# RWKV-like attention, gated MLP and a routed MLP in one kernel: the weighing of a token's own value is moved from GpSimd to VectorE and ScalarE

## The reference, cut to what matters

```python
# attention: batch 4, 8 heads, 768 tokens, head size 48
for t in range(S):
    cur = einsum('bhd,bhe->bhde', u * k[t], v[t])          # the token's own contribution, weight u
    y[:, :, t] = einsum('bhd,bhde->bhe', r[t], state + cur)
    state = w * state + einsum('bhd,bhe->bhde', k[t], v[t])
x = y as (3072 tokens, 384)
# first MLP
h = x @ w_in                                               # 384 -> 2048
g = where(h >= 1, h, where(h <= -1, 0, (h + 1) ** 2 / 4))
x = g @ w_out                                              # 2048 -> 384
# routed MLP: 8 experts, 384 -> 1024 -> 384, top 1 by cosine logits
```

## Time and profile before

| | |
|---|---|
| median of 3 runs | 806.8 us (805.24 to 806.94) |
| profiled execution | 806.01 us, span 804.3 us |
| PE busy | 739.9 us, 92% of the span |
| DVE busy | 425.6 us, 53% |
| ACT busy | 304.3 us, 38% |
| POOL busy | 149.6 us, 19% |

### The profile page before, as it was taken

The page is one execution under the profiler, slowest core; times in us unless marked ns, Lnnn a source line. Parts: engine busy times, 40 slices in busy tenths (PEclk is TensorE's granted clock), DMA queues, the critical chain, the costliest instruction groups (busy, mean ns, idle before and its releaser), DMA issues. The chain is left out here.

```text
span 804.3 us, 12788 instructions
## 1 busy us (share of the span) xinstructions
PE 739.9 (92%) x4978; PEld 619.3 (77%) x4979; DVE 425.6 (53%) x677; ACT 304.3 (38%) x505; POOL 149.6 (19%) x170
## 2 busy tenths in 40 slices
PE   3789898999999999999999999999359999999995
PEld 2668687788877887788878888888249999998985
DVE  6778765575647565475746564544354323223232
ACT  2546443543445343544444443644233212122120
POOL 7433531222222211122222200000060000000000
PEclk9999988999999999999999999999769999999998
DMA  8792110211121111111110000000360202202021
GB/s 150 197 226 48 20 30 11 70 30 21 30 69 31 31 30 22 59 30 31 28 43 1 1 1 30 11 1 1 106 212 1 79 0 79 79 1 78 0 78 39
DMA packets 88316, 40.36 MB, mean 50 GB/s; under 512 B 77112, under 2 KB 84928, under 8 KB 88256
## 3 DMA queue, kind: packets, MB, share of 16 engines
q1 hardware_dynamic: 86800, 34.61, 17.2%
q10 hardware_dynamic: 1456, 4.93, 1.6%
HBM read 30.10 MB, written 9.44 MB: 49 GB/s over the span
## 5 line engine op out<-in xcount | busy, mean ns | idle before, releaser
L856 PE MATMUL x_ps<-g_p,wout_hi 128*128 128x512 f32 x576 | 186.7, 405 | 3.5 <-DVE g_p L672 3.4
L870 PE MATMUL h_ps<-x0T,win_hi 128*128 128x512 f32 x576 | 180.1, 394 | 1.2 <-DVE x0T L601 1.2
L472 ACT ACTIVATE above<-h_ps,minus_one 128x512 f32<-128x512 f32 x96 | 65.9, 687 | 196.4 <-DVE mid L681 196.4
L681 DVE TENSOR_SCALAR mid<-h_ps 128x512 f32<-128x512 f32 x96 | 66.2, 690 | 124.7 <-PE h_ps L870 124.5
L856 PEld LDWEIGHTS x_ps<-g_p,wout_hi 128*128 128x128 f32 x576 | 104.4, 190 | 32.3 <-DVE g_p L672 6.5
L870 PEld LDWEIGHTS h_ps<-x0T,win_hi 128*128 128x128 f32 x576 | 107.5, 189 | 24.4 <-DVE x0T L601 1.5
L1401 PE MATMUL ch_ps<-x_p,w_p 128*128 128x512 f32 x432 | 109.2, 400 | 11.9 <-DVE w_p L1467 11.9
L685 DVE TENSOR_TENSOR mid<-mid,above 128x512 f32<-128x512 f32 x96 | 82.6, 861 | 70.0 <-ACT mid L473 70.0
L856 PE MATMUL x_ps<-g_p,wout_lo 128*128 128x512 f32 x288 | 113.2, 393 | 0.0
L870 PE MATMUL h_ps<-x0T,win_lo 128*128 128x512 f32 x288 | 112.6, 391 | 0.0
L1390 PE MATMUL cy_ps<-w_p,h_p 128*128 128x384 f32 x576 | 107.7, 336 | 0.0
(11 more groups left out here) (208 smaller groups left out, 652.1 us busy)
## 6 DMA issues: line engine op xcount, KB each, us to landing
xr<-xT_scratch SPq DMA_DIRECT2D x8, 768.0 KB, 4.7
rkv<-in_r SPq DMA_DIRECT2D x24, 192.0 KB, 3.0
rkv<-in_k SPq DMA_DIRECT2D x24, 192.0 KB, 3.4
rkv<-in_v SPq DMA_DIRECT2D x24, 192.0 KB, 2.8
xT_scratch<-xbuf ACTq DMA_DIRECT2D x6, 768.0 KB, 3.3
out<-acc SPq DMA_DIRECT2D x12, 384.0 KB, 2.4
win_raw<-in_moe_w_in SPq DMA_DIRECT2D x48, 64.0 KB, 2.7
wout_raw<-in_moe_w_out SPq DMA_DIRECT2D x4, 768.0 KB, 6.3
```

The source lines that it names most:

```text
L472: raises(act.activation(above[:, f % 2], h_ps[f % 2][:, :], ACT.Relu, bias=minus_one[:, :]), "over")
L681: raises(dve.tensor_scalar(mid[:, f % NM], h_ps[f % 2][:, :], -1.0, 1.0, ALU.max, ALU.min), "clamped")
L856: last = pe.matmul(x_ps[kk][:, :], (wout_hi, wout_lo)[a][:, f, cols], g_p[:, f % NG, b], start=(f == 0 and n == 0), stop=(f == NF1 - 1 and ...
L870: last = pe.matmul(h_ps[f % 2][:, :], (win_hi, win_lo)[a][:, f // QF, kk, cols], x0T[:, c % 2, b, kk], start=(kk == 0 and n == 0), stop=(k ...
```

## The change

For tiles 4 to 23 the two products of `own_weight` are issued by DVE, between `scale_k` and `own_sum`, and the diagonals by ACT, as 8 copies of 128x128 for each tile in place of one POOL instruction of 128x1024. Four of the 8 copies stand behind `g_hi` at f % 4 = 3 of the step before the tile's first, the other four behind `g_hi` at f % 4 = 0. For tile 4 all eight stand behind `g_hi` of step 0 of chunk 0. POOL keeps the copies of v and its three subtractions of weights, with nothing ahead of them but the copies of v.

```diff
         def diagonal_here(eng, it):
-            if it in (1, 3):
-                wait(eng, "diag_act", it // 2)
+            if it in (0, 2):
+                wait(eng, "diag_done", it // 2)
             elif it >= 0:
-                wait(eng, "diag_done", it // 2 if it < B else it - 2)
+                wait(eng, "diag_act", it // 2 if it < B else it - 2)
+        def own_products(eng, it, to):
+            src = rkv[:, it % B]
+            raises(eng.tensor_tensor(to[:, :, :], src[:, 0], u_rep[:, :, :], ALU.mult), "ru_done")
+            wait(eng, "ru_done", it)
+            raises(eng.tensor_tensor(to[:, :, :], to[:, :, :], src[:, 1], ALU.mult), "ruk_done")
...
                 for it in range(B, NTILE):
-                    own_weight(it, ruk)
                     rest_of_v(it, vz[:, it % 2])
-                    own_diagonal(it)
                     if it == B + 2:
...
-                def own_diagonal(it):
+                def own_diagonal(it, heads=range(H)):
                     wait(act, "q_ready", it)
-                    for h in range(H):
-                        last = act.activation(first[it].sc_m[:, h], ident[:, :], ACT.Copy, scale=q[:, it, h:h + 1])
-                    raises(last, "diag_act")
+                    if it >= B:
+                        wait(act, "y_done", it - 1)
+                    for h in heads:
+                        last = act.activation(tile_set(it).sc_m[:, h], ident[:, :], ACT.Copy, scale=q[:, it % B, h:h + 1])
+                    if H - 1 in heads:
+                        raises(last, "diag_act")
...
                         raises(act.activation(g_p[:, f % NG, 0], mid[:, f % NM], ACT.Copy), "g_hi")
+                        if attn and f % 4 == 0:
+                            own_diagonal(it, range(H // 2 if f or c else 0, H))
+                        if f % 4 == 3 and it + 1 < NTILE:
+                            own_diagonal(it + 1, range(H // 2))
                         if c == 0 and f == 1:
                             split_win(1)
...
+                def own_weight(it):
+                    rk_here(dve, it)
+                    wait(dve, "q_ready", it - 1)
+                    own_products(dve, it, ruk)
...
                 scale_k(B)
+                own_weight(B)
                 own_sum(B)
...
                             scale_k(it + 1)
+                            own_weight(it + 1)
                             own_sum(it + 1)
```

More of the change, by code:

```diff
@@ L350, in own_weight @@
                     rk_here(pool, it)
-                    if it >= B:
-                        wait(pool, "q_ready", it - 1)
-                    src = rkv[:, it % B]
-                    raises(pool.tensor_tensor(to[:, :, :], src[:, 0], u_rep[:, :, :], ALU.mult), "ru_done")
-                    wait(pool, "ru_done", it)
-                    raises(pool.tensor_tensor(to[:, :, :], to[:, :, :], src[:, 1], ALU.mult), "ruk_done")
+                    own_products(pool, it, to)
                 def rest_of_v(it, dst):
@@ L369, in own_diagonal @@
                     wait(pool, "q_ready", it)
-                    if it >= B:
-                        wait(pool, "y_done", it - 1)
                     raises(pool.tensor_tensor(tile_set(it).sc_m[:, :, :],
```

## The result

| | before | after |
|---|---|---|
| median (lowest to highest) | 806.0 us (805.0 to 806.9, 4 runs) | 815.2 us (811.8 to 818.6, 4 runs) |
| profiled execution | 806.01 us, span 804.3 | 811.77 us, span 810.0 |
| PE / DVE / ACT / POOL busy | 739.9 / 425.6 / 304.3 / 149.6 us | 736.8 / 422.7 / 348.3 / 59.2 us |

The ratio is 1.0125, 95% interval 1.0081 to 1.0169: slower by 9.2 us, forecast +9.8 (816.6, within the range). In what follows a "fall" is a drop of TensorE's granted clock from 1.00 towards 0.50. A window of 4 us that shows a value between them is a mean over both.

What follows compares the result with a forecast made beforehand. PE was taken as almost full and setting the end, so only its waits count. Terms 4.7 + 3.6 + 1.8 + 0.2 gave +10.3 on 806.01, so 816.3, plus 0.3: 816.6 us, range 811 to 821.

Steps and rivals of the forecast that it cites:

- Term 1: End of chunks 0 to 3: the last down waits longer for DVE's low part, +1.17 us four times, +4.7.
- Term 2: First tile of chunks 1 to 4: ACT's second four copies delay above and the update, +0.91 us four times, +3.6.
- Term 3: Steps 3 to 5 of chunks 1 to 4: kT comes late for the scores, +0.45 us four times, +1.8.
- Term 4: Chunk 0: four pieces and a half-counted kept clock, sum +0.2 us, between -3.5 and +4.
- Steps 0 and 1: Chunk 0: lateness of 1.17 us and 8 copies fill ACT's idle time around g_hi, +0.3 to +0.5 us.
- Step 4: Chunk 0: like Term 3, but a weight piece's split stands in place of the square, +1.3 us.
- The race: Chunk 0: POOL's first subtraction against DVE's state update; +1.3 us if POOL first, -0.2 if DVE, middle +0.5.
- The third wait: Chunk 0: wait of 3.16 us splits into two of about 1.3; g_sum earlier -0.5, half a kept clock -1.5.
- Rival A: With POOL silent, chunk 0's long waits shrink and TensorE keeps its clock, -12.8 us there: 803.3; 5%.
- Rival B: Only the chunk's end counts, ACT's copies fit its idle time, terms 2 and 3 near zero: 811.3 us; 13%.
- Rival C: Chunk 0 goes badly: POOL wins, clock falls all three times and another, +4 to +7: 821 to 823 us; 12%.
- Rival D: Longer waits at chunk starts lower the clock in each of four chunks, 3 us each: 828.6 us; 5%.

Runs made afterwards that it cites:

- e4: The changed kernel run once more, unaltered: 815.4 us, ratio 1.0127.
- e1: The kernel before with only the two products of tiles 4 to 23 moved to DVE, diagonals left on POOL: 814.3 us, ratio 1.0113.
- e3: The changed kernel with DVE taking the low part of step 15 ahead of the scaling, products and q: 809.9 us, ratio 1.0054.
- e2: The changed kernel with the two products given back to POOL, so only the diagonals are moved, to ACT: 801.3 us, ratio 0.9955.
- e9: The changed kernel with ACT's square of step 3 put ahead of the four copies of that step, chunks 1 to 5: 816.3 us, ratio 1.0134.
- e5: The changed kernel with POOL's first subtraction in chunk 0 held until DVE's low part of tile 5's rows is done: 814.3 us, ratio 1.0127.
- e6: The changed kernel with two more DVE products in step 15, lengthening the wait at chunk ends: 822.6 us, ratio 1.0228.
- e8: e2 with the low part first in step 15 and the second four copies of a chunk's first tile moved behind ACT's output copies: 797.6 us, ratio 0.9907.
- e7: The kernel before with DVE taking the low part of step 15 ahead of the scaling and q: 802.3 us, ratio 0.9971.
- e10: e8 with DVE's q ahead of the low part, all eight copies in step 15, and e5's wait on POOL: 796.8 us, ratio 0.9908.

## Why the prediction was right, and where it was not

**Direction and size: right.** +10.3 was summed, +9.2 is the difference of the medians (+10.2 in e4). The forecast's own kind held: only places where PE waits for DVE or ACT count, and there the queue's order decides.

**Term 1: right, shown.** 1.19 us for 1.17. e1 has it alone; e3 takes it away.

**Term 2: right, shown.** 0.87 for 0.91. It is absent in e1 and present in e2.

**Term 3: right in place and cause, 0.36 for 0.45.** e9 takes it away. That steps 8 and 12 cost nothing held: there is no row of PE for kT there in a full chunk.

**Term 4, chunk 0: the pieces nearly right, one thing missing.** Forecast +0.2, measured -2.7 and -1.4 (e4). By stretches, from the start of one of PE's groups to that of the next:

| stretch | forecast | before | after | e4 |
|---|---|---|---|---|
| first h to the update of step 2 | +0.3 to +0.5 | 12.75 | 13.08 | 13.05 |
| to the update of step 6 | +1.3 | 23.39 | 22.82 | 25.73 |
| to the update of step 10 | +0.5 | 25.21 | 26.55 | 26.60 |
| to the transposes of step 12 | 0 | 13.88 | 12.59 | 12.62 |
| to the update of step 14 | -2.0 | 17.02 | 14.51 | 12.90 |
| to the chunk's end, without its wait | 0 | 11.08 | 11.07 | 11.07 |

- Steps 0 and 1: right, +0.3. In e4 the waits there are 1.43 for kT (0.26 before) and 2.67 for the masked scores (3.57). In after the second is 1.43 only because the clock fell at 44 us, between the two, and slow products of PE filled the time; in e4 it fell behind both.
- Step 4: right in cause, the new wait for kT of 1.18. Its stretch depends on the fall behind the update of step 2: 22.8 us where none came there, 24.4 with a short one (e5, e6, e9; before has a short one too), 25.7 with a long one (e3, e4). At like clock that is +1.0.
- The race: I took the middle of winning and losing. POOL won it, and in the traces of e2, e3, e4, e6, e8 and e9 too (the state's update 3.87 or 3.88). That cost +1.3, which is what I had for this case. But it came not at the scores but as 1.74 us for ks at step 8, 1.2 of which e5 gave back.
- The second long wait: not in my working. It went from 3.67 to 3.00, and the stretch at 0.50 behind it was half as long: -1.3.
- The third wait split, as I had replayed, into 1.32 and 0.66 (I had 1.3 twice), and the clock came back sooner (one window at 0.59, then 0.99, for 0.50 and 0.71), or did not fall at all (e4).

The five profiles with this chunk 0 took 100.6 (after), 102.0 (e3, e4), 102.2 (e9) and 103.7 us (e6), the two with that of before 103.3 and 102.3 (e7). So -2.7 is a lucky execution, and about -0.7 is what the change is worth there (an estimate, the difference of the means).

What I missed behind these is the sign of each half. I replayed the two edits together and so never saw that the diagonals alone, off POOL's queue, are a gain of 8.2 us in chunk 0, and that the products give 5.5 to 8.6 of it back. Rival A (the freed DVE pays, 803.3) was true of one half of the change: e2 reads 801.3.

**The prologue: not foreseen.** -2.2 us in the profile, half of it the change. One cause is a row: DVE's eight small operations for w_step ran beside POOL's products for tile 4 before, and alone after. Before, then after:
```profile
27.32 1.01 POOL L354 TENSOR_TENSOR ruk<-rkv,u_rep 128x384 f32<-128x384 f32 x1 [0.76 <-DVE q L572]
...
27.56 2.79 DVE L650 TENSOR_SCALAR w_step<-ones,wcol 64x48 f32<-64x48 f32 x8
```
```profile
26.24 1.51 DVE L659 TENSOR_SCALAR w_step<-ones,wcol 64x48 f32<-64x48 f32 x8
```
That is 1.3 us of DVE. From the first update of tile 1 (27.33 before, 26.20 after) to the first h took 10.57 or 10.58 us in all seven profiles with the products on DVE, and with them on POOL 11.63 to 11.65 in three, 10.90 in e2, and 13.4 in the two in which the clock fell there (e7, e10). So 1.1 us is the products' leaving POOL, a gain that I had left out. The other 1.1 us is the moment at which PE's products in the prologue became fast. It comes at a different time from profile to profile. The windows of the prologue show a granted clock of 1.00 throughout in both kernels, so it is read from durations. Four transposes before, and the same four after:
```profile
18.27 1.06 PE L729 MATMUL a_ps<-ident,ks 128*128 128x128 f32 x4
```
```profile
18.20 0.66 PE L740 MATMUL a_ps<-ident,ks 128*128 128x128 f32 x4
```
From PE's first transposes of tile 0 to that update took 10.58 to 13.39 us over all the profiles, in no order of where the products are made.

**Rival B** (only the chunk's end counts) fell: the update waits 1.49. **Rival C** fell with chunk 0. **Rival D** was half right, and I had priced it wrongly, at 3 us in each of four chunks. A fall comes after about half of the waits of 1.95, costs 1.6 and makes a good part of the kernel's spread. With 11 of 20 it is on average 4 x 0.55 x 1.6 = 3.5 us, an estimate from these counts. My +10.3 left this out, and it left out the gains of chunk 0 and the prologue: errors of opposite sign that partly cancel, so the closeness of 816.6 to 815.2 is in part luck. The rivals' times also stand on bases that differ (806.0 under A, 806.4 under B, 806.3 under the forecast); by at most 0.4 us, this decides nothing.

## What to carry to other kernels

Price work that moves to another engine by what stands behind it in that queue at the places where the bound engine waits, not by the engine's load: here 1.2 us of products cost all of it at a chunk's end, and an order that puts the awaited operation first gets it back. Run a change of two halves as halves, because one may pay for the other: the diagonals on ScalarE were a gain, the products on DVE the loss. And when an operation is made earlier, look for what it releases: q ahead of the low part let POOL in 0.08 us early, and one more wait on POOL was worth 3 us.

## What the runs showed of the hardware

**In these traces GpSimd and VectorE exclude each other by who starts first.** A DVE operation with two SBUF inputs took 3.88 us for 0.56 beside a POOL subtraction that started 0.04 us earlier, and 1.47 for 0.68 beside a product 0.08 us earlier. The Trainium skill, "SBUF — State Buffer", section "Who interferes with whom", says that whichever issues first holds the shared ports for its whole instruction; the traces agree. The same section says that a VectorE instruction with at most one SBUF input outside the fast two-port modes doesn't contend, and counts `tensor_scalar` among those that can enter such a mode. The w_step operations have one tensor input and a scalar that is read per partition, and took 2.79 and 2.22 us (e2) beside POOL and 1.51 without it: they may run in such a mode, or the scalar may count as an input; no run here tells which.

**Whether TensorE's clock falls after a wait differs between executions of one kernel.** It fell after one of four 1.95 us waits at chunk ends in one execution of the kernel after and after three in another. The granted clock there goes between two levels, 1.00 and 0.50 of 2.4 GHz (2.4 and 1.2 GHz). After chunk ends with 0.93 us or less it fell in 0 of 28, after 1.94 or 1.95 in 11 of 20. The Trainium skill, "TensorE: Matmul & The Clock Gate", "Part 1: The HAM clock gate", says that the chip's watch on the engine runs free of the kernel, so that one kernel shows different numbers of slow products from run to run. That agrees with the counts here, and with the prologue, where the same four transposes took 1.06 us before and 0.66 after.
